# Handing an MLP over to eight experts: other order of products, loads and fetches at the seam

## The chip, the cores and the metric

One core of a Trainium2 chip runs the whole program. The metric is the device time of one execution in microseconds (us); for the kernel before it is 1026.61 us, the median of three runs (1026.44 to 1027.81).

## What is computed

Attention over chunks of 32 queries, an MLP with a rational function between its two products, and a mixture of eight experts in which each token goes to the one expert with the highest logit:

```python
# attention: q, k, v are [4, 8, 768, 64]; each chunk of 32 queries sees 8 memory keys
# and the keys from 16 before the chunk to 8 behind it; x is then [3072, 512]
h = x @ w_in                                   # 512 -> 2048
P = a[0] + a[1] * h + a[2] * h**2 + a[3] * h**3
Q = 1.0 + np.abs(b[0]) * np.abs(h) + np.abs(b[1]) * h**2
x = (P / (Q + 1e-06)) @ w_out                  # 2048 -> 512
logits = x @ w_gate                            # 512 -> 8
expert_idx = np.argmax(logits, axis=1)
gate_w = probs[np.arange(N), expert_idx]       # softmax of the logits
for e in range(8):
    mask = expert_idx == e
    out[mask] = gate_w[mask, None] * (np.maximum(x[mask] @ w1[e], 0.0) @ w2[e])
```

w1[e] is 512 x 1024, w2[e] is 1024 x 512.

## The kernel before

There are three stages. Attention fills the first part of the execution. The MLP then runs over six blocks of 512 tokens, each in 16 steps of 128 hidden columns. The experts come last and work on tiles of 128 tokens. Every product is made three times, of high and low parts (`fp32r`), which is why most loops over matmuls have the pairs (hi, hi), (hi, lo), (lo, hi): a product of one tile with half of a layer takes 12 matmuls of 512 columns or 24 for the whole layer.

**Routing.** For each block, the tokens' rows (512 numbers, a gate and a token number) are scattered by indirect DMAs of GpSimd (POOL) into a tensor in HBM that is sorted by expert, `rows_by_expert`. Tiles of one expert are then fetched back from it into `pad_rows` (which is `xg` here). The first expert is chosen early, from the counts of the first blocks, so its weights are loaded and split, and its tiles 0 and 1 fetched, while the last block of the MLP still runs.

**The seam.** Behind the last MLP step TensorE (PE) does this, in this order: the transposes of tile 0's hidden values (`transpose_h(0)`, L533), the transposes of the last block's four groups of 128 tokens (L720), their logits (L728: 32 narrow matmuls with 8 columns), two quarters of tile 1's first product (`half_product`, L540), the ranks of the last tokens within their expert (L737 to L744, they wait for `last_hot`), the rest of tile 1's first product, tile 0's second product (`second_product`, L549) with tile 1's transposes in its middle, and tile 1's second product, in which five of the eight parts stand ahead of the transposes of tile 2 (L526). Then come the first product of tile 2, the transposes of tile 3, and the loop over the tiles from 2 on: transposes of h, first product of the next tile, transposes of the tile behind that, second product of this tile.

**VectorE (DVE)** turns the logits into one-hot rows (`all_hot`, L1186), then gates (L1188 to L1192), then places for the scatter (L1195 to L1198), reads the counts (L1209 and L1210), takes the number of the first expert into a register (L1211, a register load), and works out the whole schedule of the tiles in about 30 small operations (L1214 to L1266). The last of them raises `sched_ready`. Behind it stand the low part of h of tile 1 (`lower_h`, L1053), `finish(t)` (L1061 and L1065: y of tile t times its gate into `y_sb`; it waits for `idx_s_copied`), `lower_x` (L1046), and `split_expert` (L1159), which makes the low part of each of an expert's eight weight chunks. ScalarE (ACT) makes the high parts (`upper_h` L846, `upper_x` L840, `split_expert` L836) and the relu (L851). All queues are in order.

**POOL** sends the four scatters (`send_rows`, L1301), waits until they have landed, and then goes through `fetch(t)` and `send_y(t)` in turn. `fetch(t)` waits for tile t - 1, copies that tile's gates and token numbers into `meta` (L1316), waits for its transposes and issues the DMA (L1319). `send_y(t)` copies the token numbers into `idx_s` (L1369), waits for y, scatters it into `out` (L1373) and waits for the landing. After `fetch(4)` comes a drain (L1387), and in the loop there is one behind each fetch (L1391).

**SyncE (SP)** loads the weights of the experts in eight chunks of 512 KB. For the second expert it waits until tile 2 has landed (`gathered` 48) and for `sched_ready`, and uses the buffers `x_raw` and seven of `e_raw`; chunks 6 and 7 wait for tile 1's second product, since h of tile 1 lies in their buffers. For each later expert it waits per chunk until the same chunk of the expert before has been split (L491).

## Time and profile before

| | |
|---|---|
| median of three runs | 1026.61 us |
| the profiled execution's own time | 1028.64 us |
| its span, from the first to the last instruction | 1027.0 us |
| matmuls on TensorE | 97% of the span |
| weight loads on TensorE | 80% |
| VectorE / ScalarE / GpSimd | 63% / 57% / 39% |
| mean granted TensorE clock | 0.994 of full speed |

Busy time of TensorE's matmuls is near the whole span, so the profile is read for the places where it is not busy or runs at half clock. All times that are given as a position (for example 704.9 us) count from the start of the span.

### The profile page before, as it was taken

To read this page: it belongs to the slowest core of one execution; us is meant where nothing else is said; L and a number is where in the kernel's file an instruction comes from. 1 tells how busy PE (TensorE), PEld (TensorE's weight loads), DVE (VectorE), ACT (ScalarE), POOL (GpSimd) and SP (SyncE) were. 2 spreads that over 40 slices of the span, in tenths; PEclk is the share of its full clock that TensorE was granted. 3 is DMA by queue.
4 is the path that set the end of the run, shared out by engine and by line. 5 is a ranking of instruction groups with operands and counts; after the bars stand their busy time and mean duration, and the time that the engine had idled before them with its cause. 6 is when DMAs were issued, how large, how long until landed. Compare 5 with 4: busy or idle time off the path is not lost.

```text
span 1027.0 us, 19832 instructions
## 1 busy us (share of the span) xinstructions
PE 999.0 (97%) x6222; PEld 818.5 (80%) x6223; DVE 647.8 (63%) x1211; ACT 583.8 (57%) x1255; POOL 403.4 (39%) x393
## 2 busy tenths in 40 slices
PE   7988999999999999999999999998999999999998
PEld 5766778888888888888888888886788888888886
DVE  5877788878876886787778788855224424225221
ACT  7877778766776676677666776724124324225221
POOL 3676354444544554455445546621111111112111
PEclk9999999999999999999999999989999999999999
DMA  8999613940890194059001202119112412411111
GB/s 308 347 410 353 261 42 114 363 140 12 273 347 28 62 359 153 4 188 300 0 10 41 103 21 73 42 44 350 69 41 67 174 50 83 152 41 41 32 51 36
DMA packets 58272, 143.26 MB, mean 139 GB/s; under 512 B 4711, under 2 KB 10471, under 8 KB 58224
## 3 DMA queue, kind: packets, MB, share of 16 engines
q1 hardware_dynamic: 51424, 121.07, 33.3%
q0 software_dynamic: 6800, 21.56, 6.2%
q8 instruction: 28, 0.46, 0.2%
q14 instruction: 20, 0.16, 0.0%
HBM read 71.08 MB, written 72.32 MB: 140 GB/s over the span
## 4 chain that ended last, share of the span: by engine, by line
PE 88%; ACT 3%; DMA 3%; DVE 2%; issue 2%; SPq 1%; POOL 0%; POOLq 0%; ACTq 0%; DVEq 0%
PE PS L667 25%; PE PS L509 25%; PE PS L540 14%; PE PS L549 14%; ACT prob L815 2%; PE PS L533 2%; PE PS L687 2%; PE PS L611 1%; PE PS L526 1%; DVE PS L997 1%; DMA out<-y_sb,idx_s 1%; DMA qk<-qk_all 1%; PE PS L707 1%; PE PS L581 1%; DMA pad_rows<-rows_by_expert 1%
## 5 line engine op out<-in xcount | busy, mean ns | idle before, releaser
L509 PE MATMUL PS<-xs,weights 128*128 (+1 forms) x1152 | 282.7, 394 | 0.0
L509 PEld LDWEIGHTS PS<-xs,weights 128*128 128x128 f32 x1152 | 212.7, 188 | 43.1
L667 PE MATMUL PS<-weights,g_hi 128*128 128x512 f32 x768 | 238.0, 391 | 1.3 <-POOL g_lo L1342 0.8
L1342 POOL TENSOR_TENSOR g_lo<-g_sb,g_hi 128x512 fp32r<-128x512 f32 x96 | 124.3, 1295 | 275.2 <-ACT g_hi L895 275.2
L667 PEld LDWEIGHTS PS<-weights,g_hi 128*128 128x128 f32 x768 | 143.0, 188 | 35.0 <-issue 2.9
L667 PE MATMUL PS<-weights,g_lo 128*128 128x512 f32 x384 | 149.6, 390 | 0.0
L876 ACT ACTIVATE b_ln<-PS,cf 128x512 f32<-128x512 f32 x96 | 66.0, 687 | 141.6 <-PE PS L509 141.6
L540 PE MATMUL PS<-weights,xg_hi 128*128 (+1 forms) x448 | 143.0, 401 | 0.5 <-issue 0.5
L549 PE MATMUL PS<-weights,h_hi 128*128 (+1 forms) x432 | 135.8, 395 | 1.3 <-issue 1.3
L1345 POOL TENSOR_TENSOR den<-den,b_r 128x512 f32<-128x512 f32 x96 | 128.9, 1343 | 2.1 <-ACT b_r L903 2.1
L1046 DVE TENSOR_TENSOR xg_lo<-PS,xg_hi 128x512 fp32r<-128x512 f32 x29 | 20.0, 690 | 127.3 <-ACT xg_hi L840 127.3
L540 PEld LDWEIGHTS PS<-weights,xg_hi 128*128 128x128 f32 x448 | 83.7, 192 | 17.8 <-issue 1.6
L1099 DVE SCALAR_TENSOR_TENSOR den<-den,b_r 128x512 f32<-128x512 f32 x96 | 65.9, 686 | 48.9 <-POOL den L1345 48.8
L851 ACT ACTIVATE h_sb<-PS 128x1024 f32<-128x1024 f32 x28 | 28.6, 1023 | 117.1 <-PE PS L540 117.1
L549 PEld LDWEIGHTS PS<-weights,h_hi 128*128 128x128 f32 x432 | 79.1, 188 | 16.8 <-issue 1.5
L846 ACT ACTIVATE h_hi<-PS 128x512 fp32r<-128x512 f32 x54 | 29.3, 595 | 111.1 <-PE PS L533 111.1
L540 PE MATMUL PS<-weights,xg_lo 128*128 (+1 forms) x224 | 88.6, 396 | 0.0
L549 PE MATMUL PS<-weights,h_lo 128*128 (+1 forms) x216 | 84.5, 391 | 0.0
L667 PEld LDWEIGHTS PS<-weights,g_lo 128*128 128x128 f32 x384 | 72.1, 188 | 15.1
L1108 DVE SCALAR_TENSOR_TENSOR den<-b_ln,b_r 128x512 f32<-128x512 f32 x96 | 66.1, 688 | 24.2 <-ACT b_r L879 22.6
L1065 DVE TENSOR_SCALAR y_sb<-PS,gate_s 128x512 f32<-128x512 f32 x27 | 20.3, 751 | 87.6 <-PE PS L549 75.6
L882 ACT ACTIVATE num<-PS,neg_a 128x512 f32<-128x512 f32 x96 | 74.9, 780 | 0.0
(189 smaller groups left out, 1584.7 us busy)
## 6 DMA issues: line engine op xcount, KB each, us to landing
rows_by_expert<-pad_rows SPq DMA_DIRECT2D x16, 1799.0 KB, 20.4
e_raw<-w_exp SPq DMA_DIRECT2D x34, 512.0 KB, 6.5
qk<-qk_all SPq DMA_DIRECT2D x32, 480.0 KB, 7.0
rows_by_expert<-pad_rows SPq DMA_DIRECT2D x8, 1542.0 KB, 20.0
vw<-v_all SPq DMA_DIRECT2D x32, 384.0 KB, 6.7
rows_by_expert<-pad_rows SPq DMA_DIRECT2D x8, 1285.0 KB, 17.7
w_raw<-w_mlp SPq DMA_DIRECT2D x16, 512.0 KB, 8.5
pad_rows<-rows_by_expert POOLq DMA_DIRECT2D x30, 257.0 KB, 3.0
```

Of the source, the lines that this page charges most:

```text
L509: last = pe.matmul(PS[:, H_BANK + f % 2, :], w[:, wp], rhs, start=k == 0, stop=k == 3 * KT - 1)
L540: last = pe.matmul(PS[:, half, :], xp[:, kt, :], w_half(off, kt, wp, half), start=kt == 0 and k == 0, stop=kt == KT - 1 and k == 2, skip_g ...
L549: last = pe.matmul(PS[:, y_bank(t), :], hp[:, ft, :], w_half(off, KT + ft // 2, wp, ft % 2), start=ft == 0 and k == 0, stop=ft == EKT - 1 ...
L667: last = pe.matmul(PS[:, ACC_BANK + s, :], gp[:, f % 2, s * P:(s + 1) * P], w[:, wp], start=f == 0 and k == 0, stop=f == FT - 1 and k == 2)
L846: act.activation(hi[:, 4 * c:4 * c + 4].rearrange("p k t -> p (k t)"), PS[:, h_banks(t)[c], :], ACT.Copy).then_inc(h_hi_done, 1)
L851: act.activation(h_sb[:], PS[:, 0:2, :].rearrange("p a n -> p (a n)"), ACT.Relu).then_inc(relu_done, 1)
L876: act.activation(b1_ln[:], PS[:, hb, :], ACT.Abs, scale=cf[:, 4:5]).then_inc(b12_done, 1)
L882: act.activation(num[:, par], PS[:, hb, :], ACT.Identity, scale=neg_a[:, 3:4], bias=neg_a[:, 2:3]).then_inc(u_done, 1)
L1099: dve.scalar_tensor_tensor(den[:, q], den[:, q], -2.0, b2_r0[:, q], ALU.add, ALU.mult).then_inc(w_done, 1)
L1108: dve.scalar_tensor_tensor(den[:, par], b1_ln[:], 1.0 + 1e-6, b2_r0[:, par], ALU.add, ALU.add).then_inc(q_ready, 1)
L1342: pool.tensor_tensor(g_lo[:, q], g_sb[:], g_hi[:, q].bitcast(F32), ALU.subtract).then_inc(g_lo_done, 1)
L1345: pool.tensor_tensor(den[:, st.m % 2], den[:, st.m % 2], b2_r0[:, st.m % 2], ALU.mult).then_inc(t_ready, 1)
```

## The change

On **PE** the transposes and logits of the last block are taken apart, and the quarters of tile 1's first product are put between them. Here is what stands in PE's row around the logits, in the kernel before; `PS<-cst,x` are the transposes, `PS<-wg_sb,all_t` the logits, `xg_hi`/`xg_lo` the products of tile 1:

```order
L720 MATMUL PS<-cst,x 128x128 [waits acc_dve]
L720 MATMUL PS<-cst,x 128x128 x3
L728 MATMUL PS<-wg_sb,all_t 128x8 [waits last_t_act]
L728 MATMUL PS<-wg_sb,all_t 128x8 x3
L728 MATMUL PS<-wg_sb,all_t 128x8 [waits last_t_dve]
L728 MATMUL PS<-wg_sb,all_t 128x8 x3
...
L540 MATMUL PS<-weights,xg_hi 128x512 x2
L540 MATMUL PS<-weights,xg_lo 128x512
L540 MATMUL PS<-weights,xg_hi 128x512 x2
L540 MATMUL PS<-weights,xg_lo 128x512
L737 MATMUL PS<-all_hot,tri 128x8 [waits last_hot,seen_done]
```

And in the changed kernel:

```order
L740 MATMUL PS<-wg_sb,all_t 128x8 [waits last_t_dve]
L740 MATMUL PS<-wg_sb,all_t 128x8 x3
L548 MATMUL PS<-weights,xg_hi 128x512 x2
L548 MATMUL PS<-weights,xg_lo 128x512
L740 MATMUL PS<-wg_sb,all_t 128x8 [waits last_t_act]
L740 MATMUL PS<-wg_sb,all_t 128x8 x3
L548 MATMUL PS<-weights,xg_hi 128x512 x2
L548 MATMUL PS<-weights,xg_lo 128x512
L740 MATMUL PS<-wg_sb,all_t 128x8 [waits last_t_dve]
L740 MATMUL PS<-wg_sb,all_t 128x8 x3
L548 MATMUL PS<-weights,xg_hi 128x512 x2
L548 MATMUL PS<-weights,xg_lo 128x512
```

Four quarters (12 products) now stand ahead of the last group of logits and one behind it, where before all logits came first and two quarters behind them.

On **DVE** the register load of the first expert moves from behind the reading of the counts to behind the one-hot rows:

```order
L1213 TENSOR_TENSOR all_hot<-cst,all_one 128x32 [waits last_chain]
L345 TENSOR_LOAD sched
L345 ISA x2
L1216 TENSOR_SCALAR x<-cst 128x4
L1218 TENSOR_REDUCE all_one<-all 128x4 [waits last_exp]
L1219 TENSOR_SCALAR all_one<-all_one 128x4 [waits last_chain]
L1220 RECIPROCAL x<-all_one 128x4 [waits last_chain]
L1223 TENSOR_TENSOR all<-PS,cst 128x32 [waits last_rank]
```

The load now precedes the gates and the places. The small operations of the schedule are ordered so that the list of experts comes first and raises a semaphore of its own, `list_ready`; the number of operations is the same. Behind the schedule, `split_expert` of the second expert is cut into chunk 0, chunks 1 to 3 and chunks 4 to 7. `finish(1)` (its y is the second row here) now stands behind the low parts of tile 3 and ahead of chunks 4 to 7:

```order
L1186 TENSOR_TENSOR weights<-x_raw,weights 128x1024 [waits e_hi_done]
L1072 TENSOR_TENSOR xg_lo<-PS,xg_hi 128x512 [waits xg_hi_done]
L1186 TENSOR_TENSOR weights<-e_raw,weights 128x1024 [waits e_hi_done] x3
L1072 TENSOR_TENSOR xg_lo<-PS,xg_hi 128x512 [waits xg_hi_done]
L1087 COPY gate_s<-meta 128x1 [waits y_done,meta_copied]
L1091 TENSOR_SCALAR y_sb<-PS,gate_s 128x512 [waits idx_s_copied,gate_copied,w2e_done]
L1186 TENSOR_TENSOR weights<-e_raw,weights 128x1024 [waits e_hi_done] x2
```

On **POOL**, tile 1's meta copy and tile 0's index copy stand ahead of the scatters of the rows, and the fetches of tiles 3 and 4 stand ahead of the landing of tile 0's y and of everything of tile 1's y. The rows of the changed kernel from tile 2's fetch on:

```order
L1348 DMA pad_rows<-rows_by_expert 128x514
L1407 DMA out<-y_sb,idx_s 3072x512 [waits idx_s_copied,y_done]
...
L1341 COPY meta<-pad_rows 128x2 [waits gathered]
L1348 ISA [waits tx_done,meta_copied]
L1348 DMA pad_rows<-rows_by_expert 128x514
...
L1341 COPY meta<-pad_rows 128x2 [waits gathered]
L1348 ISA [waits tx_done,meta_copied]
L1348 DMA pad_rows<-rows_by_expert 128x514
L345 TENSOR_LOAD sched
L345 ISA x2
L1400 CAST idx_s<-meta 128x1 [waits y_stored]
L1407 DMA out<-y_sb,idx_s 3072x512 [waits idx_s_copied,y_done]
```

The index copy of tile 1 (L1400), which stood between the fetches of tiles 3 and 4, now stands behind the fetch of tile 4 and the drain. On **SP** the second expert's chunk 0 needs `list_ready` alone, chunks 1 to 5 need tile 2 landed, and chunks 6 and 7 go into the buffers of chunks 0 and 1 (`second_buffer`) once these are split. The loads of each later expert start when all eight chunks of the expert before are split. The diff, cut (the reordered schedule operations and the repetitions left out):

```diff
@@ sync
             sp.wait_ge(h_ready, STEPS)
-            sp.wait_ge(gathered, 48)
+            sp.wait_ge(list_ready, 1)
+            e = load_sched(sp, R_EXP, 1, 0, E - 1)
+            for c in range(WCH):
+                if c == 1:
+                    sp.wait_ge(gathered, 48)
+                if c >= WCH - 2:
+                    sp.wait_ge(e_lo_done, upto(e_lo_done, c + 3))
+                sp.dma_start(second_buffer(c), w_exp[bass.ds(e, 1), c]...).then_inc(eraw_in[c], 16)
             sp.wait_ge(sched_ready, 1)
...
-                        sp.wait_ge(e_lo_done, upto(e_lo_done, k * WCH + (c + 1 - WCH)))
+                        if c == 0:
+                            sp.wait_ge(e_lo_done, upto(e_lo_done, k * WCH))
@@ tensor
-            half_product(0, 0, (0, 1))
+            transpose_last(0)
+            transpose_last(2)
+            half_product(0, 0, (0,))
+            transpose_last(1)
+            transpose_last(3)
+            logits_last(0)
+            half_product(0, 0, (1,))
+            logits_last(2)
+            half_product(0, 0, (2,))
+            logits_last(1)
+            half_product(0, 0, (3,))
+            logits_last(3).then_inc(last_logits, 1)
+            half_product(0, 1, (0,))
...
-            half_product(0, 0, (2, 3))
-            half_product(0, 1).then_inc(w1e_done, 1)
+            half_product(0, 1, (1, 2, 3)).then_inc(w1e_done, 1)
...
-            second_product(1, 0, range(0, 5))
+            second_product(1, 0, range(0, 4))
             transpose_x(2)
-            second_product(1, 0, range(5, EKT)).then_inc(w2e_done, 1)
+            second_product(1, 0, range(4, 6))
...
             first_product(2)
             transpose_x(3)
+            second_product(1, 0, range(6, EKT)).then_inc(w2e_done, 1)
@@ scalar
             relu(1)
-            upper_h(1)
-            upper_x(2)
-
             act.wait_ge(sched_ready, 1)
             tiles = load_sched(act, R_CNT, 0, NSUB, NSUB + E - 1)
-            split_expert(1, range(0, 5))
+            upper_h(1)
+            split_expert(1, range(0, 1))
+            upper_x(2)
+            split_expert(1, range(1, 4))
             relu(2)
             upper_x(3)
-            split_expert(1, range(5, WCH))
+            split_expert(1, range(4, WCH))
@@ vector
+            dve.wait_ge(sched_ready, 1)
+            tiles = load_sched(dve, R_CNT, 0, NSUB, NSUB + E - 1)
             lower_h(1)
             finish(0)
+            split_expert(1, range(0, 1))
             lower_x(2)
-            tiles = load_sched(dve, R_CNT, 0, NSUB, NSUB + E - 1)
+            split_expert(1, range(1, 4))
+            lower_x(3)
             finish(1)
-            split_expert(1, range(0, 5))
-            lower_x(3)
-            split_expert(1, range(5, WCH))
+            split_expert(1, range(4, WCH))
@@ gpsimd
+            keep_meta(1)
+            copy_idx(0)
             pool.wait_ge(last_rows, 1)
             for s in range(SUBS):
                 send_rows(s)
             pool.wait_ge(sched_ready, 1)
+            col = col_of(2)
             pool.wait_ge(rows_sent, upto(rows_sent, 64 * BLOCKS))
-            fetch(2, col_of(2))
+            load_tile(2, col)
             send_y(0)
-            fetch(3, col_of(3))
-            send_y(1)
-            fetch(4, col_of(4))
+            col = col_of(3)
+            fetch(3, col)
+            col = col_of(4)
+            fetch(4, col)
             pool.drain()
             tiles = load_sched(pool, R_CNT, 0, NSUB, NSUB + E - 1)
+            land_y(0)
+            copy_idx(1)
+            send_y(1)
+            land_y(1)
```

`load_tile(t)` is the DMA of `fetch(t)`, `keep_meta(t)` its meta copy, `copy_idx(t)` and `land_y(t)` are the first and the last step of what `send_y(t)` was.

## Rows read from the trace of the kernel before

**Rows 1.** The page: busy time, share of the span and instructions of TensorE's two rows.
```profile
PE 999.0 (97%) x6222; PEld 818.5 (80%) x6223; DVE 647.8 (63%) x1211; ACT 583.8 (57%) x1255; POOL 403.4 (39%) x393
```
**Rows 2.** Waits of TensorE from 700 us on: total us, times, longest.
```profile
PE PS L526 <- DMA pad_rows<-rows_by_expert: 3.4, 2, 2.3
PE PS L533 <- ACT h_sb L851: 1.6, 1, 1.6
PE PS L549 <- issue: 1.3, 1, 1.3
```
**Rows 3.** Chain of waits, in the loop: start us, length us, what.
```profile
745.50 5.48 PE PS L549 x24
...
757.75 5.48 PE PS L549 x24
```
**Rows 4.** TensorE in order of time: start us, busy us, what [idle before, releaser].
```profile
674.32 3.98 PE L728 MATMUL PS<-wg_sb,all_t 128*128 128x8 f32 x32
678.14 1.20 PE L540 MATMUL PS<-weights,xg_hi 128*128 128x512 f32 x2
...
705.97 0.66 PE L526 MATMUL PS<-cst,pad_rows 128*128 128x128 f32 x4 [1.10 <-DMA pad_rows<-rows_by_expert]
708.24 1.96 PE L533 MATMUL PS<-cst,h_sb 128*128 128x128 f32 x8 [1.62 <-ACT h_sb L851]
...
718.81 0.66 PE L526 MATMUL PS<-cst,pad_rows 128*128 128x128 f32 x4 [2.25 <-DMA pad_rows<-rows_by_expert]
720.74 0.72 PE L549 MATMUL PS<-weights,h_hi 128*128 x2 [1.26 <-issue]
```
**Rows 5.** Stretches of 2 us; behind the five busy times: granted clock, DMA share, GB/s.
```profile
676.00:678.00 2.00, 2.00 (x18) 2.00 (x17) 0.48 (x1) 0.00 (x0) 0.00 (x0) 0.86 0.00 0
...
708.00:710.00 2.00, 1.76 (x8) 1.56 (x8) 1.57 (x3) 2.00 (x4) 0.42 (x1) 0.54 1.04 422
710.00:712.00 2.00, 2.00 (x6) 1.50 (x6) 2.00 (x3) 1.97 (x4) 1.31 (x2) 0.60 1.02 418
```
**Rows 6.** VectorE in order of time, around the logits, the schedule and tile 1.
```profile
679.23 0.19 DVE L1186 TENSOR_TENSOR all_hot<-cst,all_one 128x32 bf16<-128x32 f32 x1
...
681.60 0.19 DVE L1195 TENSOR_TENSOR all<-PS,cst 128x32 f32<-128x32 f32 x1 [1.54 <-PE PS L744]
...
683.40 0.17 DVE L1214 COPY per<-twice 128x8 f32 x1 [0.82 <-DVE twice L1210]
...
688.37 0.17 DVE L1266 TENSOR_TENSOR sched<-per 128x8 int32<-128x8 f32 x1
690.96 1.29 DVE L1053 TENSOR_TENSOR h_lo<-PS,h_hi 128x512 fp32r<-128x512 f32 x2 [2.42 <-ACT h_hi L846]
...
700.63 0.75 DVE L1065 TENSOR_SCALAR y_sb<-PS,gate_s 128x512 f32<-128x512 f32 x1 [1.76 <-POOL idx_s L1369]
701.30 1.22 DVE L1159 TENSOR_TENSOR weights<-x_raw,weights 128x1024 fp32r<-128x1024 f32 x1
```
**Rows 7.** GpSimd in order of time, the fetches of tiles 2, 3 and 4.
```profile
691.73 0.59 POOL L1319 DMA_DIRECT2D pad_rows<-rows_by_expert  x1 [0.70 <-POOL meta L1316]
...
699.72 0.58 POOL L1319 DMA_DIRECT2D pad_rows<-rows_by_expert  x1 [0.69 <-POOL meta L1316]
...
711.54 0.58 POOL L1319 DMA_DIRECT2D pad_rows<-rows_by_expert  x1 [0.69 <-POOL meta L1316]
```
**Rows 8.** SyncE's issues, in order of time: start us, length us of the group, what.
```profile
696.14 0.34 SPq L486 DMA_DIRECT2D x_raw<-w_exp  x1
...
702.69 0.34 SPq L492 DMA_DIRECT2D x_raw<-w_exp  x1
703.95 9.61 SPq L492 DMA_DIRECT2D e_raw<-w_exp  x7
```
**Rows 9.** GpSimd's drains, before the loop and in it: duration ns min/median/max.
```profile
L1387 POOLq DRAIN  x1: 8742/8742/8742, 711.5 to 711.5; - x1
...
L1391 POOLq DRAIN  x25: 2979/3100/6339, 723.0 to 1017.2; - x25
```

More of the change, by code:

```diff
@@ L713, in _, with transpose_last @@
             transpose_h(0)
-            for s in LAST_ORDER:
+            def transpose_last(s):
                 if s < 2:
@@ L1214, in _ @@
             chain(dve.tensor_copy(cnt, twice[:].rearrange("p a e -> p (a e)")[:, bass.ds(first, E)]))
+            chain.ran(dve.memset(one8, 1.0))
+            n_some = chain.ran(dve.tensor_scalar(some, cnt, 0.0, None, ALU.is_gt))
             n_gt = chain.ran(dve.tensor_tensor(gt[:], cnt.unsqueeze(2).to_broadcast([P, E, SLOTS]),
                                                cst[:, C_J:C_J + SLOTS].unsqueeze(1).to_broadcast([P, E, SLOTS]), ALU.is_gt))
-            chain.ran(dve.memset(one8, 1.0))
@@ L1224, in _ @@
             chain.need(n_fill)
             n_cum = chain.ran(dve.tensor_tensor_scan(cum, one8, fill, 0.0, ALU.mult, ALU.add))
-            n_leap = chain.ran(dve.tensor_tensor(jwrap, leap[:], fill, ALU.subtract))
-            chain.need(n_cum)
-            n = chain.ran(dve.tensor_tensor(ge[:, 0], over_t, over_e(cum), ALU.is_ge))
+            chain.need(n_list)
+            n_list = chain.ran(dve.tensor_reduce(jlist, ge[:, 2, 0:E], AX.X, ALU.add))
+            chain.ran(dve.tensor_tensor(jwrap, leap[:], fill, ALU.subtract))
@@ new lines, in _ @@
+            chain.need(n_list)
+            n_list = chain.ran(dve.tensor_scalar(twice[:, 0], jlist, float(E - 1), first_e[:, 0:1], ALU.min, ALU.add))
+            n_ge = chain.ran(dve.tensor_tensor(ge[:, 0], over_t, over_e(cum), ALU.is_ge))
+            chain.need(n_list)
+            n_list = chain.ran(dve.tensor_scalar(twice[:, 1], twice[:, 0], float(E), -float(E), ALU.is_ge, ALU.mult))
+            chain.need(n_ge)
+            n_col = chain.ran(dve.tensor_tensor(ge[:, 1], ge[:, 0], over_e(jwrap), ALU.mult))
@@ L1230, in _ @@
+            chain.need(n_list)
+            dve.tensor_tensor(sched[:, R_EXP, 0:E], twice[:, 0], twice[:, 1], ALU.add).then_inc(list_ready, 1)
+            n_ord = chain.ran(dve.tensor_tensor(ge[:, 2], ge[:, 0], over_e(some), ALU.mult))
             chain.ran(dve.memset(order[:, 0:1], 0.0))
-            chain.need(n)
-            n_col = chain.ran(dve.tensor_tensor(ge[:, 1], ge[:, 0], over_e(jwrap), ALU.mult))
-            n_ord = chain.ran(dve.tensor_tensor(ge[:, 2], ge[:, 0], over_e(some), ALU.mult))
@@ L1242, in _ @@
             n_ord = chain.ran(dve.tensor_scalar(order[:, 1:], row[:, 1], 1.0, ocum[:, E - 1:E], ALU.add, ALU.min))
-            n_list = chain.ran(dve.tensor_tensor(ge[:, 1, 0:E], t_row[:, 0:E].unsqueeze(2).to_broadcast([P, E, E]),
-                                                 ocum.unsqueeze(1).to_broadcast([P, E, E]), ALU.is_ge))
+            chain.ran(dve.tensor_copy(sched[:, R_CNT, 0:1], cum[:, E - 1:E]))
             chain.need(n_ord)
+            off = row[:, 4].bitcast(I32)
+            n_off = chain.ran(dve.tensor_scalar(off, order[:, 1:], -1.0, None, ALU.add))
@@ L1246, in _ @@
+            n_new = chain.ran(dve.tensor_tensor(row[:, 2], order[:, 1:], order[:, 0:TMAX], ALU.is_gt))
             chain.ran(dve.tensor_copy(sched[:, R_ORD], order[:, 1:]))
-            n_off = chain.ran(dve.tensor_scalar(sched[:, R_EXP], order[:, 1:], -1.0, None, ALU.add))
-            n_new = chain.ran(dve.tensor_tensor(row[:, 2], order[:, 1:], order[:, 0:TMAX], ALU.is_gt))
             chain.need(n_off)
-            n_off = chain.ran(dve.tensor_scalar(sched[:, R_OFF], sched[:, R_EXP], 1, 3, ALU.bitwise_and, ALU.logical_shift_left))
@@ L1259, in _ @@
             chain.need(n_new)
[L1260 to L1266 removed]
+            dve.tensor_tensor(sched[:, R_SPLIT], row[:, 3], order[:, 1:], ALU.mult).then_inc(sched_ready, 1)
```

65 lines of the change are left out of this document (34 added, 31 removed).

## The prediction

> **What bounds the kernel now.** The page comes first: TensorE's matmuls fill 97% of the span [rows 1], so time can only be won where that engine waits or where its clock is low. The waits of TensorE from 700 us on name three causes, all of them before 721 us: 3.4 us for the DMAs of tiles 3 and 4, 1.6 us for the relu of tile 2, 1.3 us of issue [rows 2]. From 720.74 us on, tile 2's second product runs, and behind it the chain of waits is an unbroken row of matmuls: one tile every 12.25 us, 24 products in 5.48 us, which is 0.228 us for a product [rows 3]. So the end of the program hangs on one number: **when tile 2's second product starts, and at which clock**. It is 720.74 us now [rows 4]. The granted clock shows the second loss. It falls at the end of the 32 narrow logits (0.86 in the stretch from 676 us), and the next pair of products takes 1.20 us where a pair at full clock takes 0.72 or less [rows 4, 5]. It falls again after 2.7 us of idling around tile 3's transposes: 0.54 and 0.60 in the two stretches from 708 us, which costs 2 x 0.46 + 2 x 0.40 = 1.7 us [rows 5].
>
> **The change, part by part.** Positions are on the time axis of the profile before.
>
> *Logits between products.* Behind tile 0's transposes (672.7 us, as the logits' row less the 16 transposes shows) come 16 transposes (1.8 us), 32 logits (3.98 us in the row, of which the last part was slow: 3.7) and now 12 products (12 x 0.228 = 2.7). The last logits end at 680.9 us instead of 678.3 [rows 4]. The clock is taken to hold, since no run of narrow matmuls is now longer than about 1 us, where it fell at the end of 4; the other case is a rival. The one-hot rows come 1.1 us behind the last logits [rows 6]: 682.0. TensorE has one more quarter (0.7 us), then idles 0.4 us, does the ranks (0.55 us), and has 9 products left: tile 1's first product ends at 684.7.
>
> *The register load on VectorE.* It cost 0.82 us behind the counts [rows 6]. Now it stands ahead of gates and places, where VectorE had waited for the ranks 1.54 us. But that wait has shrunk to about nothing: the ranks now come 0.6 us behind the one-hot rows, and the gates with the load take 0.64 + 0.82. The places start at 682.0 + 1.5 = 683.5 instead of 681.6 [rows 6], which is **1.9 us later**. The scatters and the fetch of tile 2 follow: the fetch is issued at 691.73 + 1.9 - 0.2 (the meta copy is done earlier) = 693.4. Its landing was seen 3.1 us behind the issue (SyncE, released by it, issues at 696.14 after some 1.2 us of register loads), so tile 2 lands at 696.5 [rows 7, 8].
>
> *The schedule and tile 1's h.* The schedule's operations are reordered, not fewer. It ended at 688.54; now 688.54 + 1.9 - 0.82 = 689.6 [rows 6]. The new waits put tile 1's upper and lower h behind it and a register load (0.4 to 0.8 us), so the low part is done at 692.2, as before (690.96 + 1.29). TensorE is there at 684.7 + 5.5 + 0.9 = 691.1 and idles 1.1 us. Half of tile 1's second product (12 products) ends at 695.0, tile 2 lands 1.5 us later, its transposes end at 697.0, and its x is ready 1.9 us after they start (from 718.81 to 720.74 for tile 4) [rows 4]: the first product of tile 2 runs from 698.4 to 703.9. Before it ended at 704.9 (705.97 less the wait of 1.10) [rows 4]. What the warm clock and the moved products won has shrunk to **1.0 us**.
>
> *Loads and fetches.* Tile 3's fetch is issued at 697.8, 0.8 us behind tile 2's transposes, into a queue that SyncE has just filled with chunks 1 to 6. It took 6.2 us among the chunks before (699.72 to 705.97) [rows 4, 7]; the same now gives 704.0, where TensorE arrives. Behind the transposes 6 products of tile 1 (1.4 us) cover the relu, so the wait of 1.6 us goes. Transposes of h, 24 products and tile 4's transposes end at 712.7. Tile 4's fetch is issued at 705.8, and from then only chunk 7 is on the way, since the third expert's loads (702.69 to 713.56 before [rows 8]) now wait for the whole second expert. It has landed before 712.7, so the wait of 2.25 us and the issue of 1.26 go too.
>
> *What is late next.* Tile 1's index copy now stands behind tile 4's fetch **and the drain**. A drain lasted 8.74 us there and 2.98 to 6.34 us in the loop, median 3.10 [rows 9]: it is as long as the fetch ahead of it takes to land. With one or two chunks in the way I take 4.2 us, nearer to the median. That gives 710.0; a register load and the copy make it 710.7. VectorE's `finish(1)` waits for that copy, and behind it in VectorE's row stand the splits of chunks 4 to 7 and then tile 2's low h. So: y_sb 0.75 plus its start 0.15, four splits of 1.22 us, low h 1.29 [rows 6]: 710.7 + 0.9 + 4.9 + 1.3 = 717.8. TensorE, which could start at 712.7, idles 5.1 us.
>
> *The clock.* After the idle 2.7 us of before it ran slow and lost 1.7 us; after 5.1 us I take the same 1.7. Bounds: nothing (it stayed at full speed around the 2.25 and 1.26 us of before) and 3 us (the slow stretch from 677.7 to 684 us was twice as long as that at 708) [rows 4, 5].
>
> *Loop.* A later expert's eight loads now start together when its predecessor is split, 60 us and more ahead of their use. That costs nothing: the cover is the tiles of a whole expert.
>
> **Sum.** 717.8 + 1.7 = 719.5 against 720.74: **1.2 us less**. The profiled execution took 1028.64 us for a span of 1027.0, which is 2.0 us above the median; by its own time the sum is 1027.4, and against the median 1026.6 - 1.2 = **1025.4 us**.
>
> **A rule against a row.** Tile 3's fetch took 6.2 us while chunks were on the way and about 3 us without them [rows 4, 7]. The Trainium skill (DMA: Bandwidth & Descriptors, Queues, rings and completion order) says that each DMA engine takes turns between the queues with work, packet by packet. By that a small fetch should lose little more than its own length to the loads, and an estimate from that page's fixed 2.0 us and its 436 GB/s (Anatomy of one DMA) is 3.2 us. The row speaks against it; were it so for tile 4, the drain would end about 1 us earlier, which is rival 4.
>
> **Rivals.**
> 1. *The drain runs long* (slower than before). If tile 4's fetch again meets a full queue, the drain is 8.74 us as it was [rows 9], tile 2's low h is ready at 722.3, and with the slow clock the effect is 724.0: +3.3 us, 1029.9. For it speaks that the loads up to chunk 7 keep the DMA engines at 410 GB/s until about 708 us; against it, that the third expert's loads are behind. It decides from a drain of 5.4 us on (720.74 - 1.7 - 7.1 = 711.9 for the copy).
> 2. *The clock holds, or VectorE is earlier.* The idle stretch leaves the clock up, or the drain is at its floor too: 717.8 or 716.7, thus 2.9 to 4.1 us less: around 1023.
> 3. *The clock falls in the logits all the same.* The narrow matmuls behind which it fell are all still there. Then the last logits come 1.2 us later and the whole chain of places, tile 2, tile 3 with them: 1026.6, no gain.
> 4. *Tile 4's fetch lands undisturbed.* Drain 3.1 us, low h at 716.7, slow clock: 2.3 us less, 1024.3.
>
> The change's own aim, no wait at all, would be a start at 712.7, 8.0 us less; the copy behind the drain speaks against it.
>
> **How the numbers follow.** Forecast 45% (own range 1023.8 to 1027.3, of the 45 some 10 below the bound), rival 1 12%, rival 2 18%, rival 3 17%, rival 4 8%. A run of this kernel tells 0.2%, some 2 us, from no change. Faster by more: 10 + 18 + 7 = 35%. Slower by more: 12 + 3 = 15%. The rest, 50%, is within. The range from 1022.0 to 1029.2 takes in rivals 2, 3 and 4 and reaches into rival 1; outside are the full gain and a long drain with a long slow stretch.
>
> **What would show it.** In the changed profile: the clock at 1.00 from 674 to 684 us (else rival 3); the places some 2 us later than 681.6; a TensorE wait of about 1 us for tile 1's low h and 1.5 us for tile 2's DMA; no wait for the relu; a wait of 5 us ahead of tile 2's second product, released by VectorE's low h, behind a y_sb that waited for the index copy, behind a drain of 4 us; and half clock in the stretch behind it. The forecast is wrong if VectorE splits chunks 4 to 7 without waiting for the copy, or if the wait ahead of that product is under 3 us or over 7.

## The result and the profile after

| | kernel before | changed kernel |
|---|---|---|
| median of 12 runs each, us | 1027.21 | 1030.84 |
| lowest to highest, us | 1025.51 to 1029.53 | 1029.33 to 1033.24 |
| profiled execution: own time / span, us | 1028.64 / 1027.0 | 1030.55 / 1028.9 |

The ratio is 1.0034, with a 95% interval from 1.0023 to 1.0045: the changed kernel is **3.5 us slower** (2.4 to 4.6 us). The forecast of 1025.4 us has the wrong sign, and the measured median lies outside the range, above its end of 1029.2 us.

Positions below are on each kernel's own time axis. That of the changed kernel's trace is 0.73 us earlier where the seam begins (`transpose_h(0)` at 670.93 us against 671.66). "In the axis of before" means that 0.73 us are added.

The page's row of busy times, which answers to [rows 1], shows 0.5 us more of matmuls in a span that is 1.9 us longer.
```profile
PE 999.5 (97%) x6222; PEld 816.8 (79%) x6223; DVE 646.2 (63%) x1211; ACT 583.0 (57%) x1255; POOL 403.6 (39%) x393
```
TensorE's waits from 660 us on (total us, times, longest). The relu of tile 2, the second DMA wait and the 1.3 us of issue of [rows 2] are gone; a wait for VectorE's `h_lo` stands in their place.
```profile
PE PS L557 <- DVE h_lo L1079: 6.2, 2, 4.6
PE PS L534 <- DMA pad_rows<-rows_by_expert: 1.8, 1, 1.8
PE PS L548 <- DVE xg_lo L1072: 1.4, 2, 0.9
PE PS L762 <- DVE all_hot L1213: 0.5, 1, 0.5
```
TensorE in order of time (start us, busy us, what, [idle before, releaser]): the last logits, then each place where it waited. The last row is the start of tile 2's second product, which answers to 720.74 in [rows 4].
```profile
679.07 0.95 PE L740 MATMUL PS<-wg_sb,all_t 128*128 128x8 f32 x8
679.88 0.70 PE L548 MATMUL PS<-weights,xg_hi 128*128 128x512 f32 x2
...
692.00 0.73 PE L557 MATMUL PS<-weights,h_hi 128*128 128x512 f32 x2 [1.57 <-DVE h_lo L1079]
...
696.78 0.66 PE L534 MATMUL PS<-cst,pad_rows 128*128 128x128 f32 x4 [1.77 <-DMA pad_rows<-rows_by_expert]
...
699.36 0.72 PE L548 MATMUL PS<-weights,xg_hi 128*128 x2 [0.53 <-DVE xg_lo L1072]
...
704.93 0.64 PE L534 MATMUL PS<-cst,pad_rows 128*128 128x128 f32 x4
...
709.00 0.72 PE L548 MATMUL PS<-weights,xg_hi 128*128 x2 [0.89 <-DVE xg_lo L1072]
...
714.55 0.60 PE L534 MATMUL PS<-cst,pad_rows 128*128 128x128 f32 x4
719.76 1.22 PE L557 MATMUL PS<-weights,h_hi 128*128 x2 [4.61 <-DVE h_lo L1079]
```
Stretches of 2 us; behind the five busy times stand the granted clock, the DMA share and GB/s. The clock is 1.00 through the logits (before it was 0.86 in the stretch from 676 us [rows 5] and 0.50 in the next), and half behind the new idle time. That next stretch in the kernel before:
```profile
678.00:680.00 2.00, 2.00 (x7) 1.61 (x7) 1.47 (x9) 0.23 (x1) 0.00 (x0) 0.50 0.00 0
```
And the changed kernel:
```profile
676.00:678.00 2.00, 2.00 (x18) 1.87 (x16) 0.46 (x1) 0.00 (x0) 0.00 (x0) 1.00 0.00 0
678.00:680.00 2.00, 2.00 (x16) 1.85 (x16) 0.00 (x0) 0.00 (x0) 0.00 (x0) 1.00 0.00 0
...
720.00:722.00 2.00, 2.00 (x5) 1.65 (x6) 0.17 (x2) 0.00 (x0) 0.02 (x1) 0.50 1.00 389
722.00:724.00 2.00, 2.00 (x6) 1.55 (x5) 0.00 (x0) 0.00 (x0) 0.00 (x0) 0.50 0.94 299
```
The chain of waits (start us, length us, what) shows what that cost: the 24 products of tile 2's second product took 7.92 us, those of the next tiles 5.49. The pieces of that chain do not begin at the same edge. From the first product to the next transposes it is 7.76 us (719.76 to 727.52), and was 5.57 (720.74 to 726.31), so the half clock costs **2.2 us** here.
```profile
719.76 7.92 PE PS L557 x24
728.55 5.49 PE PS L548 x24
734.48 5.49 PE PS L557 x24
```
VectorE in order of time, which answers to [rows 6]: places, end of the schedule, the `y_sb` of tile 1 that waited for the index copy, and the four splits between it and the low h that TensorE waited for.
```profile
682.56 0.16 DVE L1223 TENSOR_TENSOR all<-PS,cst 128x32 f32<-128x32 f32 x1
...
688.60 0.20 DVE L1290 TENSOR_TENSOR sched<-row,order 128x35 int32<-128x35 f32 x1
...
713.02 0.75 DVE L1091 TENSOR_SCALAR y_sb<-PS,gate_s 128x512 f32<-128x512 f32 x1 [4.85 <-POOL idx_s L1400]
713.68 2.35 DVE L1186 TENSOR_TENSOR weights<-e_raw,weights 128x1024 fp32r<-128x1024 f32 x2
715.95 1.22 DVE L1186 TENSOR_TENSOR weights<-x_raw,weights 128x1024 fp32r<-128x1024 f32 x1
717.09 1.22 DVE L1186 TENSOR_TENSOR weights<-e_raw,weights 128x1024 fp32r<-128x1024 f32 x1
718.22 1.28 DVE L1079 TENSOR_TENSOR h_lo<-PS,h_hi 128x512 fp32r<-128x512 f32 x2
```
GpSimd in order of time, which answers to [rows 7]: the last scatter of rows, the fetches of tiles 2, 3 and 4, and the index copy of tile 1; then its drain behind `fetch(4)` and those in the loop (duration ns min/median/max), which answer to [rows 9].
```profile
688.19 0.98 POOL L1327 DMA_INDIRECT rows_by_expert<-x,place  x1 [0.30 <-issue]
693.78 0.58 POOL L1348 DMA_DIRECT2D pad_rows<-rows_by_expert  x1 [4.62 <-DMA rows_by_expert<-x,place]
...
698.23 0.58 POOL L1348 DMA_DIRECT2D pad_rows<-rows_by_expert  x1 [1.25 <-PE PS L534]
...
706.30 0.57 POOL L1348 DMA_DIRECT2D pad_rows<-rows_by_expert  x1 [1.20 <-PE PS L534]
712.69 0.19 POOL L1400 CAST idx_s<-meta 128x1 uint32<-128x1 f32 x1 [5.82 <-issue]
```
```profile
L1431 POOLq DRAIN  x1: 5777/5777/5777, 706.3 to 706.3; - x1
...
L1439 POOLq DRAIN  x25: 2987/3092/6917, 719.4 to 1019.1; - x25
```
From the start of `transpose_h(0)` to that of `transpose_h(3)` it is 56.59 us now (727.52 us less 670.93), and was 54.65 (726.31 less 671.66): 1.9 us more. Every tile behind it takes 12.3 us in both. So the loss lies inside the seam, as the forecast placed it. This distance, up to `transpose_h(4)`, is called the **seam** below: 66.90 us before, 68.88 after. The timed difference is larger than that of the two profiled executions, since these do not lie at the same place among their like: that of the kernel before took 1028.64 us, 1.4 more than its median, and that of the changed kernel 1030.55, 0.3 less than its own. Executions of one kernel differ by some 4 us, so a trace tells where time went, and the ratio how much.

### The profile page after: what moved, and what is told of

It reads as the page before. It is cut to its first block, busy times and chain, and to the rows that moved or that the text cites. A ratio compares the mean times of both kernels' runs of the same rounds, so it can differ in the third digit from the quotient of the medians.

```text
span 1028.9 us, 19809 instructions
## 1 busy us (share of the span) xinstructions
PE 999.5 (97%) x6222; PEld 816.8 (79%) x6223; DVE 646.2 (63%) x1211; ACT 583.0 (57%) x1255; POOL 403.6 (39%) x393
## 4 chain that ended last, share of the span: by engine, by line
PE 88%; ACT 4%; DVE 4%; issue 3%; DMA 1%; POOL 1%; POOLq 0%; DVEq 0%; ACTq 0%
PE PS L517 25%; PE PS L675 25%; PE PS L548 14%; PE PS L557 14%; ACT prob L840 2%; PE PS L541 2%; PE PS L695 2%; PE PS L619 1%; PE PS L534 1%; DVE PS L1023 1%; PE PS L507 1%; PE PS L589 1%; PE PS L715 1%; ACT out_t L831 0%; DMA rows_by_expert<-x,place 0%
## 5 line engine op out<-in xcount | busy, mean ns | idle before, releaser
L557 PE MATMUL PS<-weights,h_hi 128*128 (+1 forms) x432 | 138.0, 401 | 6.2 <-DVE h_lo L1079 6.2
```

The lines of the kernel that those rows point to most:

```text
L557: last = pe.matmul(PS[:, y_bank(t), :], hp[:, ft, :], w_half(off, KT + ft // 2, wp, ft % 2), start=ft == 0 and k == 0, stop=ft == EKT - 1 ...
```

## The experiments

**Theory.** As the prediction has it: VectorE's `finish(1)` waits for an index copy that is queued behind GpSimd's drain, the splits and tile 2's low h stand behind it, and TensorE idles and then runs at half clock. **Rival.** The logits between products cost the time, since they make the places, the scatters and all that follows later. All ratios are to the kernel before, measured on the same chip.

**1. The copy ahead of the drain** (changed kernel, GpSimd):
```diff
             fetch(3, col)
+            land_y(0)
+            copy_idx(1)
             col = col_of(4)
             fetch(4, col)
             pool.drain()
             tiles = load_sched(pool, R_CNT, 0, NSUB, NSUB + E - 1)
-            land_y(0)
-            copy_idx(1)
             send_y(1)
```


> The changed kernel, with tile 0's landing and tile 1's index copy moved from behind the drain to ahead of tile 4's fetch. Theory (the index copy behind the drain holds VectorE's row): the copy ends near 700 us instead of 712.9, y of tile 1 follows tile 1's second product at about 708 us instead of 713.0, the splits of chunks 4 to 7 end with ScalarE's at about 712.4, tile 2's low h is ready by 713.7, TensorE does not wait for it (4.6 us before) and stays at full clock, so tile 2's second product starts near 715.1 instead of 719.76 and takes 5.5 us instead of 7.9: 7 us less than the changed kernel, some 3.5 us less than the kernel before. Rival (the loads and ScalarE's splits are what is late, the copy only seems to be): under 2 us less than the changed kernel.

Measured: 1.0021 [1.0005, 1.0037], median 1029.33 us; seam 68.99 us. The wait did go. TensorE in order of time, tile 2's second product, and then what came at tile 5:
```profile
714.75 0.72 PE L557 MATMUL PS<-weights,h_hi 128*128 x2
...
728.88 0.66 PE L534 MATMUL PS<-cst,pad_rows 128*128 128x128 f32 x4 [2.04 <-DMA pad_rows<-rows_by_expert]
731.69 1.22 PE L557 MATMUL PS<-weights,h_hi 128*128 x2 [2.15 <-DVE h_lo L1079]
```
The product starts with no wait, straight behind the transposes. All of the gain is given back one tile later, in the same two forms and with the same half clock. VectorE and GpSimd in order of time show why:
```profile
729.49 0.75 DVE L1091 TENSOR_SCALAR y_sb<-PS,gate_s 128x512 f32<-128x512 f32 x1 [12.85 <-POOL idx_s L1400]
```
```profile
713.67 1.02 POOL L1407 DMA_INDIRECT out<-y_sb,idx_s  x1 [6.96 <-issue]
722.24 0.18 POOL L1341 COPY meta<-pad_rows 128x2 f32 x1 [7.55 <-issue]
723.13 0.55 POOL L1348 DMA_DIRECT2D pad_rows<-rows_by_expert  x1 [0.71 <-POOL meta L1341]
729.16 0.19 POOL L1400 CAST idx_s<-meta 128x1 uint32 x1 [5.48 <-issue]
```
Tile 1's scatter still stands behind the drain. It is issued at 713.67, and from 713.31 us SyncE issues the third expert's eight loads, since the second expert is now split early. The scatter takes 7.5 us to land, tile 5's fetch behind it 5.7. The step on VectorE's queue holds. That 7 us would be won does not: it is 1.3 us by the two ratios, and nothing by the two traces.

**2. The splits ahead of `finish(1)`**, with the drain left alone (changed kernel, VectorE). SyncE gets a wait ahead of the third expert's loads, which the earlier splits make necessary:
```diff
             lower_x(3)
-            finish(1)
             split_expert(1, range(4, WCH))
+            finish(1)
...
             experts = load_sched(sp, R_CNT, 1, 1, E)
+            sp.wait_ge(w2e_done, upto(w2e_done, 2))
             with sp.If(experts > 2):
```


> The changed kernel, with VectorE's finish of tile 1 behind the splits of chunks 4 to 7; the later experts' loads also wait for tile 1's second product, which is long done by then. The index copy stays behind the drain. Theory (what costs is what is queued behind the waiting instruction on VectorE, not the late copy itself): the splits end near 712.4 us, y of tile 1 at 713.8, tile 2's low h at 715.1, when TensorE arrives: again 4.6 us of waiting and 2.4 us of half clock gone, 7 us less than the changed kernel. Rival (the late copy costs through the chain of scatters and fetches behind it): the time stays within 1 us of the changed kernel.

Measured: 1.0018 [1.0005, 1.0030], 1029.31 us; seam 68.12 us. Tile 2's second product waits 0.21 us and starts at 715.99, and again TensorE waits at tile 5, 1.4 us for its DMA and then 2.1 us for `h_lo`. From the other side this is the same answer as from the first run, and the 7 us expected were missed here too.

**3. Warm matmuls in the idle time** (changed kernel, TensorE; 26 matmuls of zeros into an unused bank, behind tile 4's transposes; they add nothing to any result):
```diff
+            def pe_tile(t, fill=0):
...
                 transpose_x(t + 2)
+                warm(fill)
...
+            pe_tile(2, 26)
+            with pe.Fori(3, tiles) as t:
+                pe_tile(t)
```


> The changed kernel with 26 dummy matmuls (4.2 us, into a bank that is not used then) where TensorE idles ahead of tile 2's second product; that tile is taken out of the loop for it. The wait for tile 2's low h stays. Theory (the idle stretch lets the clock fall): tile 2's second product starts at 719.8 us as before, at full clock, 5.5 us instead of 7.9: 2.4 us less than the changed kernel. Rival (the slow stretch comes from what ran before it, or the fillers delay the product): no gain or up to 1 us lost.

Measured: 1.0015 [1.0004, 1.0026], 1028.77 us; seam 66.50 us. TensorE in order of time, and the stretch in which the clock was at half before:
```profile
719.23 0.73 PE L557 MATMUL PS<-weights,h_hi 128*128 x2 [0.77 <-DVE h_lo L1082]
```
```profile
720.00:724.00 4.00, 4.00 (x19) 3.28 (x18) 0.00 (x0) 0.00 (x0) 0.00 (x0) 1.00 0.89 321
```
The product starts as late as in the changed kernel, but at full clock, and takes 5.6 us up to the next transposes at 724.82, against 7.8 in the changed kernel. The seam is 2.4 us shorter, of which 2.2 lie behind that start, and by the ratios it is 1.9 us, so the expectation was met. The rest of what the late low h costs is the idle time itself, which the fillers leave as it is.

**4. The rival: the logits between products, alone** (kernel before, TensorE):
```diff
+            transpose_last(0)
+            transpose_last(2)
+            half_product(0, 0, (0,))
+            transpose_last(1)
+            transpose_last(3)
+            logits_last(0)
+            half_product(0, 0, (1,))
+            logits_last(2)
+            half_product(0, 0, (2,))
+            logits_last(1)
+            half_product(0, 0, (3,))
+            logits_last(3).then_inc(last_logits, 1)
+            half_product(0, 1, (0,))
```


> The kernel before, with only TensorE's part around the last logits changed: products between the logits. Theory (the logits gate the whole routing chain, so products ahead of them delay it, and the warm clock is worth nothing there): last logits 2.4 us later, places, scatters and the fetch of tile 2 about 1 us later (the ranks used to wait for slow products), and tiles 3 and 4 as much, since each waits for the one before: 1 us more than the kernel before. Rival (TensorE is the bound, and the clock that holds gives back 2.7 us): 1 to 2.7 us less than the kernel before.

Measured: 1.0010 [1.0000, 1.0021], 1028.40 us; seam 66.73 us. The clock stays at 1.00 there, and what it wins is waited for at the tiles instead. TensorE in order of time:
```profile
695.83 0.66 PE L526 MATMUL PS<-cst,pad_rows 128*128 128x128 f32 x4 [1.84 <-DMA pad_rows<-rows_by_expert]
...
707.62 0.66 PE L526 MATMUL PS<-cst,pad_rows 128*128 128x128 f32 x4 [3.23 <-DMA pad_rows<-rows_by_expert]
```
This part alone costs 1.0 us by the ratio, with an interval from 0 to 2.1, and not 3.5. The rival falls as the main cause; as a part of it, it stays.

**5. The third expert's loads held back.** The first run put the loads next on the list. SyncE waits for tile 6 before it issues them, in the kernel before (late_before), in the changed kernel (late_after), and in the kernel of the first run (late_idx):
```diff
+            sp.wait_ge(gathered, 16 * 7)
             with sp.If(experts > 2):
```


> The kernel before; the loads of the third expert (4 MB) wait until tile 6 has landed, some 60 us ahead of their use. New theory (GpSimd's one chain of fetch, index copy, scatter and landing is late, and what makes it late is the third expert's loads, among which its transfers take 6 to 8 us instead of 3): tile 1's y lands near 706 us instead of 708.9, tile 4 is fetched at 708 and lands at 712 instead of 718.8, TensorE reaches its transposes at 716.6 without the waits of 2.3 and 1.3 us: 3.5 us less than the kernel before. Rival (the second expert's own loads are what crowds the queue, or the weights are needed early): less than 1 us less, or more time.

> The changed kernel, with the third expert's loads held until tile 6 has landed. Both theories: the wait of 4.6 us ahead of tile 2's second product is over before these loads begin (they start at 718.5 us), so it stays and so does the half clock behind it; from there the changed kernel has no wait that they could cause. Within 1 us of the changed kernel.

> The changed kernel with tile 1's index copy ahead of tile 4's fetch, and with the third expert's loads held until tile 6 has landed. New theory: the copy alone gained 7 us at tile 2's second product and gave nearly all of it back at tile 5 (2.0 us for its fetch, 2.15 us for tile 3's low h, and 2.2 us of half clock), because tile 1's scatter and tile 5's fetch ran among the third expert's loads. Without these tile 5 lands by 721 us, none of the three is there: 6 to 7 us less than the changed kernel, 4 us less than the kernel before. Rival (GpSimd's chain is too long by itself, 15 us a round against TensorE's 12.3, whatever the loads do): the waits at tile 5 stay, no more than 2 us less than the copy alone.

Measured: late_before 0.9999 [0.9982, 1.0016], where 3.5 us less were expected (in its trace the waits for tile 4 are gone and the seam is 63.22 us, but the times do not show it, see run 9); late_after 1.0024 [1.0012, 1.0037], as expected; **late_idx 0.9952 [0.9938, 0.9966]**, 1023.10 us, 4.9 us less than the kernel before. Alone on the changed kernel the wait does little: 4.68 us ahead of tile 2's second product, as without it. With the copy ahead of the drain as well, no wait is left behind tile 3. The waits of TensorE in late_idx:
```profile
PE PS L535 <- DMA pad_rows<-rows_by_expert: 1.8, 1, 1.8
PE PS L558 <- DVE h_lo L1080: 1.5, 1, 1.5
PE PS L549 <- DVE xg_lo L1073: 0.5, 1, 0.5
```
Tile 1's scatter lands in 3.1 us there, against 7.5 in the first run. Both steps are needed: the copy out from behind the drain, and the DMA chain of GpSimd out from among the loads.

**6. The register load back behind the counts** (late_idx, on VectorE, with ScalarE's `upper_h(1)` ahead of its wait for the schedule):
```diff
+            upper_h(1)
             act.wait_ge(sched_ready, 1)
...
-            first = load_sched(dve, R_CNT, 2, 0, E - 1)
...
             n = chain.ran(dve.tensor_copy(twice[:, 1], counts))
+            first = load_sched(dve, R_CNT, 2, 0, E - 1)
```


> As late_idx, and VectorE's register load stands behind the counts again, and ScalarE's upper h of tile 1 ahead of its wait for the schedule. The places come 0.8 us earlier, tile 2 lands 0.8 us earlier and with it every step up to tile 2's second product; TensorE's wait of 1.6 us for tile 1's low h shrinks, which is worth nothing by itself since tile 2 is waited for behind it. 0.8 us less than late_idx, some 5 us less than the kernel before. Rival (the loads of the second expert set the pace from tile 2 on): no difference to late_idx.

Measured: 0.9962 [0.9948, 0.9976], 1024.06 us; seam 61.12 us against 61.45. The trace is a little shorter, the time is not. The place of the load is worth less than this measurement tells.

**7. No drain at all** (changed kernel, GpSimd), a question to the drain itself:
```diff
             fetch(4, col)
-            pool.drain()
             tiles = load_sched(pool, R_CNT, 0, NSUB, NSUB + E - 1)
```


> The changed kernel without the drain behind tile 4's fetch; the one in the loop stays, and the third expert's loads start as in the changed kernel, when the second is split. Theory (the drain is what holds tile 1's index copy and scatter, and their lateness is what pushes GpSimd's chain among the third expert's loads): the copy at 707.5 us instead of 712.7, y of tile 1 at 709, its scatter lands at 713 before those loads begin near 714, tile 5's fetch is issued near 715 and has landed by 722: no wait at tile 2's second product and none at tile 5, 7 us less than the changed kernel, 4 to 5 less than the kernel before. Rival (the loads push tile 5's fetch out in any case): as with the copy alone, 2 us less than the changed kernel.

Measured: 0.9961 [0.9949, 0.9973], 1024.18 us, 4.0 us less than the kernel before and some 7.5 less than the changed one; seam 62.90 us. GpSimd in order of time:
```profile
708.96 0.57 POOL L1348 DMA_DIRECT2D pad_rows<-rows_by_expert  x1 [1.37 <-PE PS L534]
709.54 0.19 POOL L1400 CAST idx_s<-meta 128x1 uint32<-128x1 f32 x1
712.13 1.18 POOL L1407 DMA_INDIRECT out<-y_sb,idx_s  x1 [2.40 <-DVE y_sb L1091]
```
The copy follows the fetch at once. Taking out that one instruction turns the loss into a gain, which is the plainest proof of the cause. The scatter of tile 1 goes out ahead of the third expert's loads (SyncE issues them from 715.98), so they need not be held back.

**8. Chunk 0 of the second expert behind tile 2** (on the kernel of 6). In the changed kernel this load is issued at 687.15, between the scatters. Cut: SyncE and ScalarE are shown, VectorE's splits are regrouped in the same way.
```diff
-                if c == 1:
+                if c == 0:
                     sp.wait_ge(gathered, 48)
...
-            split_expert(1, range(0, 1))
             upper_x(2)
-            split_expert(1, range(1, 4))
+            split_expert(1, range(0, 4))
```


> As late_idx_reg, and chunk 0 of the second expert waits for tile 2 like chunks 1 to 5, split behind tile 2's x. Theory (chunk 0's load crowds the scatters of the last rows, which landed 4.5 to 4.9 us behind the last issue instead of 3.7): the scatters land 1 us earlier, tile 2 with them, and tile 2's first product starts 1 us earlier; the chunks come 0.5 us later, which may show as a wait at the relu of tile 2. 0.5 to 1 us less than late_idx_reg. Rival (one chunk is too little to crowd anything): the landing stays at 4.5 us, and the later chunks cost up to 1 us.

Measured: 0.9955 [0.9938, 0.9971], 1022.95 us; seam 61.94 us. GpSimd in order of time, the last scatter and the fetch of tile 2:
```profile
687.91 0.97 POOL L1326 DMA_INDIRECT rows_by_expert<-x,place  x1 [0.30 <-issue]
692.05 0.59 POOL L1347 DMA_DIRECT2D pad_rows<-rows_by_expert  x1 [3.17 <-DVE y_sb L1091]
```
The fetch goes out 4.1 us behind the issue of the last scatter, instead of 5.4 in the kernel of 6 and 5.6 in the changed one. The profile puts its wait down to `y_sb`, but `load_tile(2)` waits for the scatters alone (`rows_sent`), so it is still their landing that releases it, only earlier. The other traces say the same: the first instruction behind that wait comes 3.5 to 4.5 us behind the last issue in the six without this load, and 4.8 to 5.2 us in the eight with it. That chunk 0 crowds the scatters is confirmed. It wins nothing that these times tell, and one cost is seen: every later chunk comes later, and the relu of tile 2 waits 1.6 us.

**9. The kernel before with late loads, again** (late_before_2, the edit of 5)**, and with the logits' order** (late_logits, the edits of 4 and 5).

> late_before once more (the kernel before, third expert's loads held until tile 6 has landed): its trace was 3.7 us shorter in this part, its times did not show it. If the trace is typical, the ratio lies at 0.9965; if the gain is there in some executions alone, at 0.998 to 1.000 and with a wide spread again.

> late_before with TensorE's part around the last logits changed (products between the logits). Theory (with the third expert's loads away TensorE is nearer to being the bound, but each tile's fetch still waits for the one before, and the places come about 1 us later): 0 to 1 us more than late_before. Rival (the clock that holds now gives back its 2.7 us): 2 us less than late_before.

Measured: 0.9995 [0.9983, 1.0008], 1027.05 us, and 1.0011 [0.9999, 1.0024], 1028.80 us; seams 64.06 and 65.69 us. Once more the logits' order costs some 1.6 us on top, somewhat more than the upper end expected, and far from the whole loss. The first of the two stays unexplained in part: twice its trace has a seam 2.8 to 3.7 us shorter than that of before, and twice the time hardly moves. Most of the gap is the choice of the execution: the two profiled ones took 1025.97 and 1025.05 us, 1.3 and 2.0 less than the medians of their kernel, where that of before took 1.4 more than its own.

Its two traces showed something else. Stretches of late_before_2, in which the order of the logits is that of the kernel before:
```profile
676.00:678.00 2.00, 2.00 (x15) 1.87 (x16) 0.64 (x4) 0.23 (x1) 0.00 (x0) 1.00 0.00 0
678.00:680.00 2.00, 2.00 (x27) 1.56 (x26) 1.57 (x11) 0.00 (x0) 0.00 (x0) 1.00 0.00 0
```
The same instructions ran at 0.86 and 0.50 in the trace of before. From `transpose_h(0)` to `transpose_h(1)` it is 18.0 us there, 16.5 in late_before, 15.0 in late_before_2, and 15.7 in the trace of the changed kernel. So with one and the same order the logits are slow in one execution and not in another. How often they are slow is taken up below.

## Why the prediction was wrong

Its steps one by one, positions in the axis of before:

| step | sum | trace |
|---|---|---|
| last logits end | 680.9 | 680.8 |
| one-hot rows | 682.0 | 681.9 |
| places start | 683.5 | 683.3 |
| schedule ends | 689.6 | 689.5 |
| tile 1's low h, TensorE idle | 692.2, 1.1 | 692.7, 1.6 |
| fetch of tile 2 issued | 693.4 | 694.5 |
| tile 2 landed | 696.5 | 697.5 |
| first product of tile 2 | 698.4 to 703.9 | 700.1 to 705.7 |
| fetch of tile 3 issued, landed | 697.8, 704.0 | 699.0, 705.6 |
| fetch of tile 4 issued | 705.8 | 707.0 |
| drain | 4.2 | 5.8 |
| index copy done | 710.7 | 713.6 |
| second product of tile 2 starts | 717.8 | 720.5 |
| idle ahead of it | 5.1 | 4.6 |
| lost to half clock behind it | 1.7 | 2.2 |

**The mechanism was right.** The clock held in the logits, the places came 1.7 us later (1.9 in the sum), the relu wait and tile 4's DMA wait went, and the wait that took their place was the one named, with its releaser, its four splits and its length: from the copy to the product it took 6.9 us where the sum had 7.1. Runs 1, 2 and 7 each take away one link, the copy behind the drain, the splits behind the waiter, and the drain itself, and each time this wait is gone or down to 0.2 us.

**Three terms were too small, and all on the same path.** They are the step from the places to the fetch of tile 2, tile 3's fetch, and the drain:
- *The scatters' landing, +1.1 us.* The sum moved the fetch of tile 2 with the places and left the landing as it was. The change also puts chunk 0's load (issued at 687.15 us) between the scatters, and they landed 4.9 us behind the last issue. Run 8 takes that load away, and the fetch goes out 1.3 us sooner behind the last scatter than in the kernel that it starts from. The price of a moved step includes the transfers that it now runs beside.
- *Tile 3's fetch, +0.4 us*: it landed in 6.6 us instead of 6.2.
- *The drain, +1.6 us.* It was taken to last as long as the fetch takes to land. Tile 4's fetch landed in 4.3 us, about as assumed, but the drain lasted 5.8. The same surplus was to be had from before and was not looked up: the drain ahead of the loop had 8.74 us [rows 9] for a fetch that landed in 7.2. It does not come from the loads, and it is no property of every drain: in all fourteen traces the first drain of the execution lasted 1.4 to 1.6 us beyond the landing of its fetch, with the hardware queue full or empty (4.48 us for 3.0 in late_before), and those behind it did not (6.92 us for 6.8 at tile 5 of the changed kernel). In the run without this drain, the first one of the loop had the surplus instead: 8.75 us for a landing in 7.2. Why the first one is longer, no run tells. Run 7 shows what this one instruction costs where it stands.

Smaller differences make −0.4 us together (the fetch of tile 4 followed tile 3's landing in 1.4 us and not 1.8, the splits and low h took 6.9 and not 7.1). The start of the product is thus later than the sum by 1.1 + 0.4 + 1.6 − 0.4 = 2.7 us: 720.5, within 0.3 us of the 720.74 of before. All that the edits win ahead of it is eaten.

**The clock, +0.5 us.** The row of before had lost 1.7 us behind 2.7 us of idle time; behind 4.6 us it was 2.2 us (7.76 less 5.57), inside the stated bounds of 0 to 3. Run 3 gives it back. In the trace this slow product is the whole loss: the start is 0.2 us earlier than before, and from it to the next transposes it is 7.8 us instead of 5.6.

From the forecast of −1.2 us these make −1.2 + 2.7 + 0.5 = +2.0 us, and the traces show +1.9.

**A misread row, and a step that was not in the sum.** The 1.9 us from transposes to a ready x were read from 718.81 and 720.74 us. But the product at 720.74 is tile 2's second and reads h, not this x. VectorE's low x of tile 4, which is the last part of it, was ready only at 720.82 us, 2.0 us behind the transposes, in the kernel before:
```profile
720.13 0.69 DVE L1046 TENSOR_TENSOR xg_lo<-PS,xg_hi 128x512 fp32r<-128x512 f32 x1 [5.87 <-ACT xg_hi L840]
```
The x of tile 2 was ready 2.6 us behind its transposes, and that of tile 3 waited 0.9 us, because ScalarE's relu stood behind the split of a chunk that had come late. The first of these brought TensorE to tile 3's transposes at 705.7 us, just when that tile had landed (705.6), so there two causes bind within 0.1 us. The second lies off the path, since TensorE then waited for VectorE anyway.

**What the clock in the logits was worth.** The row of 1.20 us and the clock of 0.86 [rows 4, 5] are not there in every execution of the old order. Where the logits run at full clock in the kernel before too, the change has nothing to win there, and the later places are its price alone. But such executions do not seem to be the usual ones. The mean granted clock of the 35 executions of the kernel before that were timed beside runs 1 to 4 has a median of 0.994 (0.989 to 0.997), and the profiled one had 0.994 as well; the 12 of run 4, which differ in the order of the logits alone, have 0.9955. An estimate from these two: 0.0015 of 1027 us, 1.5 us of clock won in the mean. Run 4 is 1.0 us slower in spite of it, since what is won there is waited for at the tiles.

**The rivals.** What happened has the place and the sign of rival 1, but not its reason. The drain was 5.8 us, over the 5.4 from which it was said to decide, and by that sum it would have cost 0.4 us; the rest is the late fetches ahead of it and the clock. Rival 1 had the fetch meet a full queue, and was given 12% with the argument that the third expert's loads are behind. That argument held: the fetch landed in 4.3 us. What was missing is the drain's own surplus. Rivals 2 and 4 fell (drain 5.8 us, half clock behind the wait), and so did 3 (clock 1.00 in the logits). Fetches landed in about 3.0 us with the hardware queue empty, and in 5.7 to 8.0 us among the loads. The Trainium skill (DMA: Bandwidth & Descriptors, Queues, rings and completion order) has the DMA engines take turns between queues packet by packet, and from that and the figures of its section Anatomy of one DMA came the estimate of 3.2 us for a fetch among loads; these traces do not agree with that estimate either.

## What to carry to other kernels

Before an instruction is queued behind a drain, list who waits for it, and what stands behind the waiter on its own engine: here a 0.2 us index copy held four splits and a low part, and so the bound engine, for 4.6 us. Price such a drain by its own row and not by the transfer ahead of it, above all the first of the execution. When a wait is taken away, look one period further: what the faster engine sets free (the next loads) may meet the transfers that the next tile needs, and here the moved copy and the later loads gave 4.9 us only together. Taking out the drain gave 4.0 us by itself.

## What the runs showed of the hardware that was not expected

- The first drain of an execution lasted 1.4 to 1.6 us longer than the landing of the fetch ahead of it, in all fourteen traces: 5.78 against 4.3 us in the changed kernel, 8.74 against 7.2 before, 4.48 against 3.0 in late_before. Those behind it ended with the landing, within 0.2 us (about 3.1 us in the loop, and 6.92 against 6.8 among loads).
- A fetch of 257 KB on the software queue lands in about 3.0 us alone and in 5.7 to 8.0 us beside a filled hardware queue (5.7 in idx_ahead, 8.0 in logits_alone); a scatter of y in 3.1 us (late_idx) or 7.5 us (idx_ahead). One load of 512 KB beside four scatters put off the fetch behind them by 1.3 us (5.4 us behind the last scatter in the kernel of 6, 4.1 without the load).
- The granted clock at the same instructions differs from one execution to the next: 0.50, 0.87 and 1.00 in the 2 us from 678 us, in the traces of before, late_before and late_before_2, which have the same order of the logits.
- After 4.6 us of idling the 24 products took 7.76 us up to the next transposes, at a granted clock of 0.50 in the stretches from 718 to 724 us; with matmuls of zeros in that time, and 0.8 us of idling left, they ran at full clock (5.59 us, 5.57 in the kernel before).
